# Token product batch by batch, with theta of batch 1 between its blocks

## The reference

```python
theta = x @ w_theta                              # x: (2, 768, 512)
zr = x * np.cos(theta)
zi = x * np.sin(theta)
yr = np.einsum('ts,bsd->btd', w_tok_r, zr)       # 768 x 768 over the positions
yi = np.einsum('ts,bsd->btd', w_tok_i, zi)
u = x + yr + yi
x = u + np.maximum(u @ w_ch, 0.0)
```

## Time and profile before

| what | value |
|---|---|
| median of 3 executions | 495.57 (494.82 to 501.33) |
| time of the profiled execution | 494.67 |
| its span | 492.7 |
| TensorE busy | 454.3 (92%) |
| VectorE busy | 252.8 (51%) |
| GpSimd busy | 218.8 (44%) |
| ScalarE busy | 159.8 (32%) |
| mean granted clock of TensorE | 0.978 of full speed |

### The profile page before, as it was taken

How to read it: one execution, slowest core, us unless ns; L and a number is a source line. 1 busy time by engine, 2 the same in 40 slices (tenths; PEclk the granted TensorE clock), 3 DMA queues, 4 the chain that set the end, 5 groups by cost and what they waited for, 6 DMA issues and landing times.

```text
span 492.7 us, 7401 instructions
## 1 busy us (share of the span) xinstructions
PE 454.3 (92%) x2640; PEld 397.7 (81%) x2640; DVE 252.8 (51%) x509; ACT 159.8 (32%) x392; POOL 218.8 (44%) x162
## 2 busy tenths in 40 slices
PE   0999999999979956999999999699999999999997
PEld 0678788888868735999999998488788779999885
DVE  4698888988754999600000035871532321333322
ACT  2345554455632746321111123331422230111121
POOL 1589777797000557654444223830000037444342
PEclk9999999999997979899999999899999999999999
DMA  5453355431000000042000002410000200000122
GB/s 189 168 169 102 87 152 168 129 108 37 1 2 5 0 0 1 1 153 104 0 0 0 0 0 65 126 34 1 0 1 0 85 0 0 1 0 0 64 91 100
DMA packets 10219, 26.43 MB, mean 54 GB/s; under 512 B 1360, under 2 KB 1872, under 8 KB 10192
## 3 DMA queue, kind: packets, MB, share of 16 engines
q1 hardware_dynamic: 8848, 20.85, 13.5%
q0 software_dynamic: 1344, 5.24, 2.9%
HBM read 22.94 MB, written 3.15 MB: 53 GB/s over the span
## 4 chain that ended last, share of the span: by engine, by line
PE 78%; DVE 15%; ACT 2%; issue 2%; DMA 1%; POOL 1%; SPq 0%; DVEq 0%; ACTq 0%; POOLq 0%
PE ps L1066 18%; PE ps L1067 18%; PE ps L1068 18%; PE ps L1118 8%; PE ps L1093 5%; PE ps L1103 4%; DVE red L950 2%; PE ps L1087 2%; PE ps L1113 2%; PE ps L1073 2%; DVE xtl L807 1%; DVE ps L953 1%; DVE red L946 1%; DVE red L956 1%; DVE den L816 1%
## 5 line engine op out<-in xcount | busy, mean ns | idle before, releaser
L1066 PE MATMUL ps<-tok_hi,zl 128*128 128x384 f32 x192 | 65.1, 339 | 4.9 <-POOL zl L492 4.9
L567 ACT ACTIVATE probs<-ps,neg_max 128x288 f32<-128x288 f32 (+2 forms) x96 | 45.9, 491 | 65.1 <-DVE neg_max L801 65.1
L1068 PE MATMUL ps<-tok_hi,zh 128*128 128x384 f32 x192 | 64.8, 338 | 0.0
L1067 PE MATMUL ps<-tok_lo,zh 128*128 128x384 f32 x192 | 64.7, 337 | 0.0
L1118 PE MATMUL ps<-v_raw,p_t 128*128 128x64 f32 x352 | 48.8, 280 | 0.0
L982 DVE TENSOR_TENSOR x_t<-ps,x_t 128x768 f32 (+1 forms) x8 | 7.7, 958 | 79.6 <-PE ps L1068 79.6
L1118 PEld LDWEIGHTS ps<-v_raw,p_t 128*128 128x128 f32 x352 | 42.9, 191 | 5.4 <-issue 1.6
L1066 PEld LDWEIGHTS ps<-tok_hi,zl 128*128 128x128 f32 x192 | 36.5, 190 | 5.6 <-issue 4.9
L801 DVE TENSOR_REDUCE neg_max<-ps 128x1 f32<-128x288 f32 (+2 forms) x96 | 36.0, 416 | 4.6 <-PE ps L1093 4.2
L1067 PEld LDWEIGHTS ps<-tok_lo,zh 128*128 128x128 f32 x192 | 36.6, 191 | 0.0
L1068 PEld LDWEIGHTS ps<-tok_hi,zh 128*128 128x128 f32 x192 | 36.5, 190 | 0.0
(11 more groups left out here) (142 smaller groups left out, 1127.3 us busy)
## 6 DMA issues: line engine op xcount, KB each, us to landing
stage<-in_w_tok SPq DMA_DIRECT2D x12, 384.0 KB, 3.2
k_raw<-in_k_t SPq DMA_DIRECT2D x8, 448.0 KB, 4.0
q_raw<-in_q_t SPq DMA_DIRECT2D x8, 384.0 KB, 3.1
v_raw<-in_v_p SPq DMA_DIRECT2D x8, 384.0 KB, 2.9
out<-o_sb SPq DMA_DIRECT2D x12, 256.0 KB, 2.0
stage<-in_w_sp SPq DMA_DIRECT2D x6, 384.0 KB, 3.3
in_raw<-in_moe_w_in POOLq DMA_DIRECT2D x1, 2048.0 KB, 8.7
th_raw<-in_moe_w_theta POOLq DMA_DIRECT2D x1, 1024.0 KB, 9.0
```

Source lines behind the costliest of these rows:

```text
L567: act.activation(probs[i % 2][:, 0:ncols(i), h], s_ps[i % 2][:, h, 0:ncols(i)], ACT.Exp, bias=neg_max[:, i % 2, h:h + 1], accum_out=sums[: ...
L1066: pe.matmul(dst, w_lo, m_hi, start=first, stop=False)
L1067: pe.matmul(dst, w_hi, m_lo, start=False, stop=False)
L1068: return pe.matmul(dst, w_hi, m_hi, start=False, stop=last)
```

## The change

Theta of pairs 1 and 2 follows pair 0 as before; then TensorE starts the token product of batch 0, and puts theta of pairs 3, 4 and 5 behind its first three blocks. The blocks of batch 1 follow those of batch 0. The lists of the other engines are written in the same order, the loops over them are unrolled, and the blocks take turns between the two PSUM banks by their number. VectorE makes the real low half of block (0,0). The loads of w_in and w_ch are issued after the last rotation, and a piece of w_ch is split behind the parts of each block of batch 1. The semaphore `s_z` of the rotated tiles is split in one for zi and one for zr.

The diff, cut to its core:

```diff
@@ gpsimd
-            with pool.Fori(0, GT // 4 - 1) as n:
-                for j in range(4):
-                    rotate(n, j)
-            for c in range(2):
-                z_low(0, 0, c)
-            for j in range(4):
-                rotate(GT // 4 - 1, j, both=False)
-            for c in range(2):
-                z_low(0, 1, c)
-            for b in range(2):
-                pool.wait_ge(s_theta[b], GT // 2)
-            pool.dma_start(in_raw[:, :, :], w_in.rearrange("(c p) n -> p c n", p=P)).then_inc(s_in_raw, 16)
-            pool.dma_start(ch_raw[:, :, :], w_ch.rearrange("(c p) n -> p c n", p=P)).then_inc(s_ch_raw, 16)
...
+            for k in range(HALVES - 1):
+                rotate(k)
+            rotate(HALVES - 1, both=False)
+            z_low(0, 0, 1)
+            for n in range(HALVES):
+                for c in range(2):
+                    z_low(0, n + 1, c)
+                rotate(HALVES + n)
             for b in range(2):
+                pool.wait_ge(s_theta[b], 2 * HALVES)
+            pool.dma_start(in_raw[:, :, :], w_in.rearrange("(c p) n -> p c n", p=P)).then_inc(s_in_raw, 16)
+            pool.dma_start(ch_raw[:, :, :], w_ch.rearrange("(c p) n -> p c n", p=P)).then_inc(s_ch_raw, 16)
+            for n in range(KC):
                 for c in range(2):
-                    z_low(KC - 1, b, c)
+                    z_low(1, n, c)
+                split_ch(n)
@@ scalar
             x_high_half(2)
-            for k in range(GT // 2 - 3):
-                x_high_half(k + 3)
-                trig_half(k)
-            trig_half(GT // 2 - 3)
-            for b in range(2):
-                act.wait_ge(s_z[b], TILES)
-            for c in range(2):
-                z_high(0, 0, c)
-            for j in range(4):
-                trig(GT // 4 - 1, j)
...
+            x_high_half(3)
+            trig(0)
+            trig(1)
+            x_high_half(4)
+            trig(2)
+            for j in range(2):
+                act.wait_ge(s_zr[j], HALVES)
+            z_high(0, 0, 0)
+            for j in range(2):
+                act.wait_ge(s_zi[j], HALVES)
+            z_high(0, 0, 1)
+            for n in range(HALVES):
+                for c in range(2):
+                    z_high(0, n + 1, c)
+                if n == 0:
+                    x_high_half(5)
+                trig(HALVES + n)
+            rotated(1)
+            for n in range(KC):
+                for c in range(2):
+                    z_high(1, n, c)
@@ vector
-            for n in range(GT // 4):
-                for half in range(2):
-                    if n < GT // 4 - 1:
-                        for b in range(2):
-                            x_low(n + 1, 2 * half + b)
-                    reduce(n, half)
...
+            x_low_half(2)
+            reduce(0)
+            reduce(1)
+            x_low_half(3)
+            reduce(2)
+            for b in range(2):
+                dve.wait_ge(s_sin[b], 2 * HALVES)
+                dve.wait_ge(s_zi[b], HALVES)
+                tile = slice(TILES - 2 + b, TILES - 1 + b)
+                dve.tensor_tensor(x_sb[:, tile, :], x_sb[:, tile, :],
+                                  cos_x[b][:, :].rearrange("p (o n) -> p o n", o=1), ALU.mult).then_inc(s_zr[b], 1)
+            x_low_half(4)
+            dve.wait_ge(s_zh[0], 1)
+            dve.tensor_tensor(zl[0][:, :, :], x_sb[:, 0:TILES, 0:P], zh[0][:, :, :].bitcast(F32),
+                              ALU.subtract).then_inc(s_zl[0], 1)
+            for n in range(HALVES):
+                add_y(0, n)
+                reduce(HALVES + n)
+                if n == 0:
+                    x_low_half(5)
+            add_y(0, KC - 1)
+            for n in range(KC - 1):
+                add_y(1, n)
             u_low(0)
-            add_y(KC - 1, 1)
+            add_y(1, KC - 1)
@@ tensor
-            for j in range(2, 4):
-                theta(0, j)
-            with pe.Fori(1, GT // 4) as n:
-                for j in range(4):
-                    pe.wait_ge(s_theta_used[j % 2], 2 * n + j // 2 - 1)
-                    theta(n, j)
...
+            def theta_half(k):
+                for b in range(2):
+                    if k >= 2:
+                        pe.wait_ge(s_theta_used[b], k - 1)
+                    theta(k // 2, 2 * (k % 2) + b)
...
+            theta_half(1)
+            theta_half(2)
             pe.wait_ge(s_wlo, 2 * TILES)
...
+            for n in range(HALVES):
+                token_block(0, n)
+                theta_half(HALVES + n)
+            token_block(0, KC - 1)
+            for n in range(KC):
+                token_block(1, n)
```

More of the change, by code:

```diff
@@ L262, in attn_moe_gmlp @@
         s_sin = [sem(f"sincos_ready{b}") for b in range(2)]
-        s_z = [sem(f"z_ready{b}") for b in range(2)]
+        s_zi = [sem(f"zi_ready{b}") for b in range(2)]
+        s_zr = [sem(f"zr_ready{b}") for b in range(2)]
         s_zh = [sem(f"zh_ready{c}") for c in range(2)]
@@ L474, in _ @@
                 x_copy(PAIRS - 1, b)
[L477 to L486, removed]
@@ L489, in z_low, with rotate @@
-            def z_low(n, b, c):
+            def rotate(k, both=True):
+                for b in range(2):
+                    pool.wait_ge(s_xcopy[b], PAIRS)
+                    pool.wait_ge(s_sin[b], 2 * k + 2)
+                    tile = slice(2 * k + b, 2 * k + b + 1)
+                    pool.tensor_tensor(zi_sb[:, tile, :], x_sb[:, tile, :],
+                                       sin_x[b][:, :].rearrange("p (o n) -> p o n", o=1), ALU.mult).then_inc(s_zi[b], 1)
+                    if both:
+                        pool.wait_ge(s_zi[b], k + 1)
+                        pool.tensor_tensor(x_sb[:, tile, :], x_sb[:, tile, :],
+                                           cos_x[b][:, :].rearrange("p (o n) -> p o n", o=1), ALU.mult).then_inc(s_zr[b], 1)
@@ L725, in chunk @@
                                    ACT.Relu).then_inc(s_hg_used, 1)
-            act.wait_ge(s_u[0], KC)
+            for p in range(2):
+                act.wait_ge(s_u[p], KC // 2)
             u_high(0)
@@ L734, in _ @@
             act.wait_ge(s_in_lo, KC)
-            act.wait_ge(s_u[1], KC)
+            for p in range(2):
+                act.wait_ge(s_u[p], KC)
             for n in range(NCHUNK - 1):
@@ L934, in _, with reduce @@
                 dve.wait_ge(s_g_theta, 1)
-            def reduce(n, half):
-                turn = 2 * n + half
+            def reduce(turn):
+                half = turn % 2
                 theta = [banks[2 + half][:, b, :] for b in range(2)]
@@ L963, in _, with x_low_half, add_y @@
                 dve.wait_ge(s_xcopy[b], PAIRS)
-            for n in range(GT // 4):
-                for half in range(2):
-                    if n < GT // 4 - 1:
-                        for b in range(2):
-                            x_low(n + 1, 2 * half + b)
-                    reduce(n, half)
-            for j in range(4):
[L972 to L981, removed]
+            def x_low_half(k):
+                for b in range(2):
+                    x_low(k // 2, 2 * (k % 2) + b)
+            def add_y(b, n):
+                turn = KC * b + n
+                dve.wait_ge(s_zused[1], turn + 1)
+                part = (slice(None), slice(n, n + 1), slice(b * SEQ, (b + 1) * SEQ))
                 dve.tensor_tensor(x_t[part].rearrange("p o (h t) -> p (o h) t", h=2),
-                                  banks[b][:, :, 0:HALFSEQ],
-                                  x_t[part].rearrange("p o (h t) -> p (o h) t", h=2), ALU.add).then_inc(s_u[b], 1)
+                                  banks[turn % 2][:, :, 0:HALFSEQ],
+                                  x_t[part].rearrange("p o (h t) -> p (o h) t", h=2), ALU.add).then_inc(s_u[turn % 2], 1)
             def u_low(n):
@@ L1237, in _, with token_block @@
-            token_block(0)
-            with pe.Fori(1, KC) as n:
-                token_block(n)
+            def theta_half(k):
+                for b in range(2):
+                    if k >= 2:
+                        pe.wait_ge(s_theta_used[b], k - 1)
+                    theta(k // 2, 2 * (k % 2) + b)
+            def token_block(b, n):
+                turn = KC * b + n
+                if turn >= 2:
+                    pe.wait_ge(s_u[turn % 2], turn // 2)
+                for c in range(2):
+                    pe.wait_ge(s_zl[c], turn + 1)
+                    for s in range(TILES):
+                        for g in range(2):
+                            cols = slice(g * HALFSEQ, (g + 1) * HALFSEQ)
+                            mm = product(banks[turn % 2][:, g, 0:HALFSEQ], zh[c][:, s, :], zl[c][:, s, :],
+                                         tok_hi[:, c * TILES + s, cols], tok_lo[:, c * TILES + s, cols],
+                                         c == 0 and s == 0, c == 1 and s == TILES - 1)
+                    mm.then_inc(s_zused[c], 1)
@@ L1251, in chunk @@
                     mm.then_inc(s_r_ps, 1)
-                pe.wait_ge(s_u[1], KC)
```

(2 more changed lines are left out.)

54 lines of the change are left out of this document (21 added, 33 removed).

## The result

| | median | lowest to highest | runs |
|---|---|---|---|
| kernel before | 496.01 | 494.82 to 501.33 | 4 |
| changed kernel | 507.45 | 506.46 to 509.04 | 4 |
| ratio | 1.021 | 95%: 1.013 to 1.029 | |
| the two timed again, against each other: before | 497.22 | 495.5 to 505.39 | 12 |
| changed | 504.79 | 503.04 to 506.72 | 6 |

A forecast was written before the change was run, and what follows sets the result against it. TensorE's own work bounds the kernel, except where it waits. 187.0 + 8 x 12.46 + 16.5 + 2.3 + 2.3 = 307.8 against 299.4 or 300.0: 8 us later, so 503, range 498 to 508.

The forecast's parts named there:

- The bound: Whole kernel: TensorE's own work sets the time except where it waits; matmuls unchanged, so the change moves only waits.
- Step 1: Chain through VectorE, ScalarE and GpSimd to the first token matmul: block (0,0) starts at 187.0 us.
- my sign of being wrong: First token matmul starting before 183 or after 190 us, or a changed length of the stage after the product.
- the first rival: At reduce(1) and reduce(2), GpSimd and VectorE hardly meet: block (0,0) starts about 182, 5 less, 497.7 us; chance 0.12.
- zl on VectorE: Ahead of block (0,0): VectorE's subtraction starts 0.5 us before GpSimd's, at no cost; coming second, block starts at 188.8.
- Step 2: Restart of TensorE after standing still 20 us: lower clock costs 2.3 us, ends 1.7 and 2.9.
- Step 3: Blocks of batch 0: parts ready at E + 13.15, wanted at E + 17.95; margin 4.8, no wait ahead of (0,1) to (0,3).
- Step 4: Into batch 1: ready at E + 14.8 against E + 12.46, a wait of 2.3 us ahead of (1,0).
- My lower bound of 0.7: Wait ahead of (1,0) if GpSimd's two DMA issues cost nothing: 0.7 us.
- Sum: End of the token product: 187.0 + 8 x 12.46 + 16.5 + 2.3 + 2.3 = 307.8, 8 us later than before.
- the 2% to which I had given 0.75: Whole kernel: time stays within about 2%, 10 us, of the kernel before; chance 0.75, slower 0.22, faster 0.03.
- the rival of longer waits: Clock falls ahead of (1,0) (1.7), w_ch split delays z_low(1,1) (1 to 2), zl second (1.8); two give 506 to 507; chance 0.25.

The follow-up runs named there:

- narrowed products: Changed kernel with GpSimd's eight products of pairs 0 and 1 covering 64 of 512 columns, a probe of the time only; 501.77 us (one execution).
- changed again: The changed kernel, unaltered, run once more for a second profile; 507.69 us (one execution).
- pair 3 ahead: Changed kernel with theta of pair 3 multiplied ahead of block (0,0), in TensorE's long wait; median 501.56 us.

## Why the prediction was right

I forecast 503 and a range of 498 to 508. The two comparisons gave 507.45 and 504.79, both inside it; the stage itself got 7.8 us longer for 8 forecast. That the first median lies inside too is in part luck: most of its 4.4 us over 503 have no term in my sum. By its steps:

- **The bound.** Right. TensorE's matmuls are the same, and its waits are 18.87 and 2.46 in place of 6.14, 4.51 and 0.41. Block (0,0) starts 39.97 - 28.46 = 11.5 us sooner, and 16.5 us of theta come behind it; the wait ahead of (1,0) adds 2.05 to the old 0.41, and the low clock at the start of the product costs 2.6 for 1.7. That is 16.5 - 11.5 + 2.05 + 0.9 = 7.95, against 7.8 measured.
- **Step 1, start of block (0,0).** I had 187.0 - 157.64 = 29.4 us behind the first range reduction; three profiles gave 28.5. (By the absolute time, 189.76, it came close to my sign of being wrong, "after 190", which took no account of the 3.7 us ahead of the stage.) Clamps and split beside GpSimd took 1.98 and 3.42 for my 2.14 and 3.48. What I had too long is reduce(2), lengthened by 1.1 and not 1.7; another 0.3 lies ahead of it. The 4.4 us that the narrowed products gave back sit close to the 5 that I had put on this contention in the first rival.
- **zl on VectorE.** It went first and took 0.95; GpSimd's started 0.6 behind it. The order that would have cost 1.8 did not occur in any profile, so its price was not tested. VectorE's zl, then GpSimd's:

```profile
188.66 0.95 DVE L1030 TENSOR_TENSOR zl<-x_sb,zh 128x768 fp32r<-128x768 f32 x1
```
```profile
189.29 2.00 POOL L496 TENSOR_TENSOR zl<-zi_sb,zh 128x768 fp32r<-128x768 f32 x1 [2.54 <-ACT zh L655]
```

- **Step 2, the clock.** The restart at the lower level cost (1 - 0.52) x 5.5 = 2.6 us, forecast 2.3.
- **Step 3.** No wait ahead of (0,1) to (0,3); 222.89 - 204.91 = 17.98 for one block and one pair, forecast 17.95.
- **Step 4.** 2.46 for 2.3, but for a reason half wrong. I let the two issues carry 1.6 of it; moving them gave 0.44, since ScalarE's high half takes most of the same time. My lower bound of 0.7 should have been near 2.
- **Sum.** 7.8 us in the stage (7.7 and 9.0 in the other two profiles) for 8 forecast. In the longer comparison that is a ratio of 1.017, within the 2% to which I had given 0.75. Of the rival of longer waits one term of three came true in one profile of three, as a clock that fell behind a wait of 2.46 us; the other two did not occur.
- **What I had not in the sum** is the spread outside the stage. I took one profiled execution's first 157 us for a constant; they run from 155.8 to 167.5. In the profiles of the first comparison this, and no term of the sum, makes the difference 12.7 instead of 7.8. Its median difference of 11.4 fits that, but no profile of its other executions shows it.

The largest thing to say about the change is its first effect. The wait that I priced at 20 us had room for two of the three pairs of theta that were put behind it. Batch order with these two pairs ahead of the first block has a stage 8 us shorter than before, not 8 longer. What the old order would gain if its own waits of 11.1 us were filled in the same way was not tried.

## What to carry to other kernels

When work is reordered so that a stage can start sooner, ask what the bounding engine does until then: work moved from ahead of the new start to behind it is paid in full, and the start must come sooner by more than that. Then put back ahead of the start whatever already has its inputs and its bank. And compare kernels by a stage between two marks of the trace: here it repeated to 0.0 to 1.3 us where whole runs spread over 10.

## What the hardware showed beside this

- A VectorE step on 128x2 elements took 4.38 us because a GpSimd instruction of 4.51 us ran beside it, and the two ended within 0.04 us of each other; it took 0.16 where none did, and 1.21 at most beside the same work in four pieces. The cost here is that of a small step in another engine's chain. The Trainium skill (SBUF — State Buffer, Who interferes with whom) says that a VectorE step of this kind (`tensor_scalar`) can need a pair of ports that it shares with GpSimd, and that whoever issues first then holds the pair for its whole instruction. The trace agrees.
- Waits of 2.46 to 2.49 us ahead of block (1,0) were followed by 3.4 us of the lower clock in two of six profiles (changed again, pair 3 ahead) and by none in four. The same wait can thus cost 2.5 us or about 4.
- TensorE's first matmuls were half as long again, 0.42 us for 0.27, until about 21 us in one execution of the kernel before and until about 28 in another. This put the second 3.4 us behind by itself.
